# Weights requested in half pieces; ScalarE and VectorE take a tile's round trip in another order

## The reference

```
a   = softmax(q k^T / 8, kept: 4 sink keys and a window of 128) v     # 2 x 8 heads, 768 tokens, head size 64
h   = x @ w_in;  y = (h - tanh(h)) @ w_out                             # 1536 tokens, 512 -> 2048 -> 512
gate: top 2 of 8 experts by x@w_gate + log1p(exp(x@w_noise)) * noise
out[token] += weight * (relu(x @ w1[e]) @ w2[e])                       # per expert 512 -> 1024 -> 512
```

## Time and profile before

| | |
|---|---|
| runs shown | 790.99, 787.76 and 791.50 us; median 790.99 |
| profiled execution, its own time | 789.29 us |
| its span (first to last instruction) | 787.4 us |
| mean granted TensorE clock | 0.977 of 2.4 GHz |
| busy share of the span | PE 95%, POOL 55%, DVE 45%, ACT 29% |
| mean DMA rate | 156 GB/s, 122.48 MB in all |

### The profile page before, as it was taken

How to read it: one execution, slowest core, us unless ns; L and a number is a source line. 1 busy time by engine, 2 the same in 40 slices (tenths; PEclk the granted TensorE clock), 3 DMA queues, 4 the chain that set the end, 5 groups by cost and what they waited for, 6 DMA issues and landing times.

```text
span 787.4 us, 12786 instructions
## 1 busy us (share of the span) xinstructions
PE 746.5 (95%) x3884; PEld 624.8 (79%) x3885; DVE 358.1 (45%) x879; ACT 229.1 (29%) x528; POOL 436.4 (55%) x240
## 2 busy tenths in 40 slices
PE   7999999999999999999987999989998989999884
PEld 6677898898989999998875887868776878888763
DVE  4777533234323523444653444444453535444425
ACT  5999522223223223322311211112111111211100
POOL 6888995000200300069699679297937887803662
PEclk9999999999999999999998999999999999999996
DMA  8542492000200100053636476757657575636748
GB/s 296 221 136 90 141 358 97 1 1 0 81 1 0 71 9 0 0 188 119 260 105 237 149 252 212 263 190 240 213 173 281 182 271 197 216 130 194 218 144 286
DMA packets 59837, 122.48 MB, mean 156 GB/s; under 512 B 6689, under 2 KB 21665, under 8 KB 59809
## 3 DMA queue, kind: packets, MB, share of 16 engines
q1 hardware_dynamic: 28128, 63.92, 22.8%
q10 hardware_dynamic: 27840, 45.62, 17.5%
q0 software_dynamic: 3840, 12.59, 4.7%
HBM read 82.26 MB, written 39.85 MB: 155 GB/s over the span
## 4 chain that ended last, share of the span: by engine, by line
PE 80%; DMA 11%; DVE 3%; issue 2%; ACT 2%; POOL 1%; ACTq 0%; DVEq 0%; POOLq 0%
PE bank L1449 17%; PE bank L1399 17%; PE bank L1542 17%; PE bank L1571 16%; DMA hid_by_lane<-hid 8%; PE bank L1352 4%; PE bank L1343 3%; DMA hid_lanes<-hid_by_lane 3%; PE bank L1325 2%; PE bank L1465 1%; DVE bank L1153 1%; DVE hid L1161 1%; PE bank L1524 1%; PE bank L1459 1%; ACT arena L739 1%
## 5 line engine op out<-in xcount | busy, mean ns | idle before, releaser
L1571 PE MATMUL bank<-ring,hidT_hi 128*128 (+1 forms) x496 | 165.1, 415 | 17.9 <-DVE hidT_lo L1174 13.7
L634 POOL TENSOR_TENSOR ring<-ring_raw,ones 128x2048 fp32r<-128x2048 f32 x32 | 116.0, 3624 | 61.9 <-DMA ring_raw<-in_moe_w 61.8
L636 POOL TENSOR_TENSOR ring<-ring_raw,ring 128x2048 fp32r<-128x2048 f32 x32 | 148.0, 4624 | 2.5
L1542 PE MATMUL bank<-ring,xsT_hi 128*128 (+1 forms) x496 | 135.6, 396 | 7.7 <-DVE hid L1161 6.7
L682 POOL DMA_INDIRECT sorted_x<-y_rows,arena x24 | 25.3, 1053 | 204.6 <-DVEq L1097 198.5
L1571 PEld LDWEIGHTS bank<-ring,hidT_hi 128*128 128x128 f32 x496 | 95.3, 197 | 41.4 <-issue 20.0
L1449 PE MATMUL bank<-w_out_sb,gated_hi 128*128 128x512 f32 x384 | 121.1, 397 | 0.0
L1542 PEld LDWEIGHTS bank<-ring,xsT_hi 128*128 128x128 f32 x496 | 94.0, 191 | 29.2 <-issue 9.5
L1571 PE MATMUL bank<-ring,hidT_lo 128*128 (+1 forms) x248 | 101.2, 408 | 0.0
L1018 DVE TENSOR_TENSOR arena<-bank,arena 128x384 f32<-128x384 f32 x64 | 35.6, 557 | 115.8 <-ACT arena L794 114.8
L1399 PE MATMUL bank<-xT_hi,w_in_hi 128*128 (+1 forms) x256 | 86.7, 339 | 0.0
(11 more groups left out here) (185 smaller groups left out, 993.4 us busy)
## 6 DMA issues: line engine op xcount, KB each, us to landing
ring_raw<-in_moe_w SPq DMA_DIRECT2D x32, 1024.0 KB, 8.4
hid_by_lane<-hid ACTq DMA_DIRECT2D x29, 512.0 KB, 3.1
hid_lanes<-hid_by_lane ACTq DMA_DIRECT2D x29, 512.0 KB, 3.4
sorted_y<-ys ACTq DMA_DIRECT2D x31, 256.0 KB, 3.8
xs<-sorted_x ACTq DMA_DIRECT2D x27, 256.0 KB, 2.8
sorted_y<-zeros SPq DMA_DIRECT2D x1, 4864.0 KB, 25.4
arena<-in_k SPq DMA_DIRECT2D x8, 520.0 KB, 4.1
w_in_raw<-in_moe_w_in SPq DMA_DIRECT2D x2, 2048.0 KB, 9.5
```

Source lines behind the costliest of these rows:

```text
L634: pool.tensor_tensor(hi, raw, one_like(raw), ALU.mult).then_inc(rounded, 1)
L636: ins = pool.tensor_tensor(lo, raw, hi.bitcast(F32), ALU.subtract)
L1542: last = pe.matmul(bank[1 + half][:, :], x[:, c * P:(c + 1) * P], ring[:, bass.ds(at * 2 * WE + (w + c * FE + half * BANK), BANK)], start= ...
L1571: last = pe.matmul(bank[5][:, :], x[:, c * P:(c + 1) * P], ring[:, bass.ds(at * 2 * WE + (w + CH * FE + c * DM), DM)], start=c == 0 and n ...
```

## The change

Four edits. (1) SP requests the first half of a piece, waits until it has landed, requests the second half and waits again; one half piece (512 KB) is under way at a time. The semaphores of the pieces count 32 instead of 16, and POOL waits for both halves. (2) ACT issues `hid_in(t)` as the last thing in `tile(t)`, behind `hid_turned_out(t - 1)` and `store_rows(t - 2)`. (3) DVE turns tile t - 1 inside `tile(t)`, behind `rows_turned_out(t + 1)`, where it had turned tile t at the end of `tile(t)`. (4) The first tiles are written out accordingly: ACT issues `hid_in(2)` behind the input work of tile 4, and DVE turns tile 2 behind the relu of tile 3. What is computed stays the same, and so do the bytes.

```diff
@@ SyncE, for experts 2 to 7
                     sp.wait_ge(used_up, n)
                     dst, src = raw_piece(e, expert, j)
-                    sp.dma_start(dst, src).then_inc(piece_loaded[e % RING][j], 16)
+                    before = 32 * (e // RING - 1)
+                    mid = dst.shape[1] // 2
+                    sp.dma_start(dst[:, 0:mid, :], src[:, 0:mid, :]).then_inc(piece_loaded[e % RING][j], 16)
+                    sp.wait_ge(piece_loaded[e % RING][j], before + 16)
+                    sp.dma_start(dst[:, mid:, :], src[:, mid:, :]).then_inc(piece_loaded[e % RING][j], 16)
+                    sp.wait_ge(piece_loaded[e % RING][j], before + 32)
@@ GpSimd
-                        pool.wait_ge(piece_loaded[e % RING][j], 16 * (e // RING))
+                        pool.wait_ge(piece_loaded[e % RING][j], 32 * (e // RING))
@@ ScalarE, first tiles
             hid_out(2, first=True)
-            hid_in(2, first=True)
             rows_turned_out(4)
             load_rows(5)
+            hid_in(2, first=True)
             relu_out(3)
@@ ScalarE, tile(t)
                     load_rows(t + 2)
-                hid_in(t)
                 hid_turned_out(t - 1, used=t)
                 store_rows(t - 2)
+                hid_in(t)
@@ VectorE, first tiles
             relu_out(2)
-            turn_hidden(2)
...
             relu_out(3, written=True)
+            turn_hidden(2)
             hid_turned_out(2)
-            turn_hidden(3)
@@ VectorE, tile(t), and the end
                 rows_turned_out(t + 1)
+                turn_hidden(t - 1)
                 result_out(t - 2)
                 hid_turned_out(t - 1)
-                turn_hidden(t)
...
+            turn_hidden(TILES - 2)
             result_out(TILES - 3)
```

## The result

The changed kernel takes 764.34 us (median of 4 runs, 762.46 to 765.27), the kernel before 790.43 in the same comparison; the ratio is 0.967, with a 95% interval of 0.964 to 0.970. The forecast was 764.5. On the chips of the later comparisons the kernel before had medians of 787.0 (beside e1 to e4), 788.0 (e5 to e8) and 786.2 us (e9 to e12): the gain was 26.1 us here and 22.4 in e11, the changed kernel once more. Lines of code are 5 higher now: L878 is ACT's relu (L873 before), L865 the write of the hidden values (L860), L873 the read-back (L868), L886 `hidT_hi` (L881), L1158 the transposes (L1153).

The account below looks back on a forecast made before the run. TensorE was taken as nearly always busy, held up when load bursts made writes late and ACT's order passed that on. Steady 17.5, start 7.0 and end 0.7 make 25.2 us: 764.1, forecast 764.5, range 760 to 776.

Parts of the forecast that it names:

- The sum: Whole kernel: gains of steady part, start and end together 25.2 us, giving 764.1 and a forecast of 764.5 us.
- steady part: Passes of the expert stage from 444.91 to 738.71 us: 18.5 us at stake, 17.5 taken as gained, bounds 0 and 18.5.
- start: Around `up(4)`: relu of tile 3 no longer behind tile 2's transposes, 7.0 us gained, bounds 4 and 7.6.
- end: Last tiles: `down(28)` follows `down(27)` at once, idle 2.35 us becomes 1.6, so 0.7 us gained.
- what the new orders do: ACT and DVE loop: with the read-back moved, a write may take 10 us or more; before, ACT fell behind from 5.
- short writes alone: Writes of `hid` beside half pieces: 4 to 6 us, which even the old order would nearly have hidden.
- the moved read-back: `hid_in(t)` issued about U + 7.5, U being the end of `up(t)`: 3.42 us, more likely 4 to 4.5.
- The loads: SP's half pieces of weights: 4.3 us each against 4.9 us free, so loads keep up and POOL is fed.
- the 12 pieces of the prediction's stretch: From the request at 498.59 to expert 6's first `up` at 637.07: 117.7 us for 24 halves, 4.9 us each.
- signs of being wrong: TensorE waiting for POOL's split, or at `up` for DVE's relu or input, or POOL waiting long for `ring_raw`.
- starve POOL: Rival, same stretch: a half takes 5.5 us, 24 take 132, 14.3 more than there is: 779 us; chance 0.08.
- make the loads the bound: Rival, first `up` of expert 6: at 6.5 us a half the loads give 803 us, slower than before; chance 0.04.

Follow-up runs that it names:

- e1: The changed kernel with whole 1 MB pieces requested as before, keeping the new ScalarE and VectorE orders: 780.5 us, ratio 0.993 to the kernel before.
- e4: The kernel before with only ScalarE's loop changed, the read-back issued behind the roundings and the store: 796.9 us, ratio 1.015 to the kernel before.
- e5: The kernel before with only VectorE's new order, in loop and first tiles; whole pieces, old ScalarE order: 778.9 us, ratio 0.986.
- e8: The changed kernel with TensorE itself turning the last tile's hidden values, without their write and read-back: 760.97 us, ratio 0.966 to the kernel before.
- e9: The changed kernel without ScalarE's part: half pieces and VectorE's new order, ScalarE's old order: 764.5 us, ratio 0.972 to the kernel before.
- e12: The changed kernel with TensorE turning the last tile's hidden values, measured again beside the changed kernel: 762.66 us, ratio 0.969 to the kernel before.
- e11: The changed kernel once more, unedited, on the chip of the last comparisons: 763.84 us, ratio 0.970 to the kernel before.
- e2: The kernel before with only half pieces requested one at a time, old ScalarE and VectorE orders: 782.0 us, ratio 0.994 to the kernel before.
- e3: The kernel before with only VectorE's first tiles edited, tile 2 turned behind the relu of tile 3: 787.45 us, ratio 1.002 to the kernel before.
- e7: The changed kernel with quarter pieces of 256 KB, one at a time: 820.29 us, ratio 1.043 to the kernel before.
- e6: The changed kernel with whole 1 MB pieces, one at a time: 768.85 us, ratio 0.975 to the kernel before.

## Why the prediction was right, and where it was not

**The sum.** The change gained 27.1 us of span. By its terms, forecast and measured: steady part 17.5 and 17.2 (18.36 less 1.14); start 7.0 and 7.35 (14.07 less 6.72); end 0.7, and 2.25 from tick 29 to tick 30 (21.22 to 18.97). The rest, 0.3, lies before the tick of tile 2 and after the last tick. Of the end, 0.7 is the shorter pause (2.35 to 1.63) as worked out; the other 1.5 us is the clock, which I had left out. After 1.63 us of pause the stretch has a granted clock of 1.00, where it had been 0.77 (747.1 to 754.4 us in the kernel before):

```profile
721.30:728.00 6.70, 6.70 (x29) 5.47 (x30) 3.32 (x4) 0.00 (x0) 6.70 (x8) 1.00 0.37 120
```

In e11 the pause is 1.94 us, the clock 0.77 in the same stretch, and the pass 1.9 us longer (20.85): this term comes and goes. That forecast and median lie 0.2 us apart is luck: the gain in span was 27.1 us against 25.2 forecast, and by medians 26.1 here and 22.4 in e11.

**The step that failed: what the new orders do.** The prediction said that ACT's order is what makes a late write TensorE's matter, that with the read-back moved a write may take 10 us or more, and that short writes alone would nearly have been hidden in the old order. The first is right and not the whole: e5 shows that wait, ahead of `down`, behind writes of 8.5 and 10.0 us. The other two are wrong. e1 has the new orders and late writes and loses 12.9 us. The prediction had taken 3.4 to 4.5 us for the moved read-back; issued into a burst it took 7.6, ACT stood for it, and the load of the input tile behind it, which the prediction does not mention, landed late for TensorE. e2 has short writes and the old orders and loses 13.7 us, in a circle that the prediction did not count: there is one `hid`, one `hid_by_lane` and one `hid_lanes`, so write, read-back, and in the old order also transposes and relu, follow one another before the next write can go out. e9 shows that ACT's move is worth nothing that could be measured beside the other two.

What the runs show in its place: VectorE's order takes the transposes and the relu, 2.9 us, out of the circle, and halves hold a write to 5.5 and a read-back to 6.2 us. With halves and the old order the circle was 13.29 us against a pass of 11.48 (e2); in the kernel before it sets the time once, from the write at 556.32 (8.54 us, read-back 3.85) to the next at 571.98. With whole pieces and the transposes out of the circle, single transfers of 7.6 to 10 us reach TensorE by whatever stands behind them in ACT's order, the rounding (e5) or the input tile (e1). The single gains in the steady part are 4.7 (e2) and 5.5 (e1), together 10.2; both at once gain 17.2. The medians say the same: 5.0 (e2) and 6.5 us (e1) against 22.4 (e11). I got the sum right because I credited the pair with everything; my reasons would have credited either alone with nearly as much.

**The start** was worked out for tile 4 alone. `up(4)` begins 1 us after `up(3)`, as forecast, in e3 too; that it stays won is the work of the halves, which the prediction did not say. With whole pieces the chain runs through the circle here: in e5 the write of 421.93 takes 8.73 and the read-back 3.27 us, and TensorE waits 2.4 us one tile later.

**The loads.** Forecast were 4.3 us a half against 4.9 free, and no wait. A half landed after 4.4 us (median), and TensorE waited all the same, 0.89 us at 616.09. The chain of the changed kernel ahead of it (start us, us, what):

```profile
563.70 5.61 PE bank L1576 x24
...
569.48 4.11 DMA ring_raw<-in_moe_w
...
582.30 5.56 DMA ring_raw<-in_moe_w
...
588.42 0.88 SPq L571
...
589.76 4.07 DMA ring_raw<-in_moe_w
...
603.10 4.26 DMA ring_raw<-in_moe_w
```

Two things that the prediction did not count stand in it. SP reads its table only behind the last wait of an expert, which takes 1.9 us from 587.86 to 589.76. And the 12 pieces of the prediction's stretch are not one stretch: from 480 to 620 us SP also waited for TensorE (total us, times, longest us):

```profile
SPq L579 <- PE bank L1576: 12.6, 2, 9.2
```

The shorter of the two, 3.4 us, ends at 569.31: pieces 2 and 3 of expert 5 can't be requested before the last `down` of expert 3 is over. What binds is therefore the four passes from there to the first `up` of expert 6, with 8 halves, the table and the last split. From the request at 569.48 to the last landing at 607.36 it is 37.9 us, and 37.0 were free; less 1.9 for the table that is 4.4 us a half, not 4.9. The halves took 4.5 each, request to request, one of them 5.6. A wait for a split ahead of an expert's first `up` is one of the signs of being wrong that the prediction listed; it cost 1.1 us. The rivals that starve POOL or make the loads the bound were given 0.08 and 0.04; their place was right, their threshold too generous, and the kernel sits on the true one: TensorE waited 0.9 and 1.0 us there in two executions (after, e9) and not in e11, and with quarters 55 us are lost in the steady part. The fit that the prediction quotes from the Trainium skill, "DMA: Bandwidth & Descriptors", section "Anatomy of one DMA", is stated there for DMAs that GpSimd issues; SP's halves took 4.4 us where the estimate from it was 3.2.

## What to carry to other kernels

When a loop passes its data through single buffers, count the circle of waits as a whole, and compare it with the pass. When an instruction is moved away from a late transfer, price what then stands behind it, every transfer in the queue included: a wait that one edit removes comes back under another name as long as the late transfer is there. Splitting a large transfer bounds what a small one beside it can wait, and spreads the load over more passes; that pays only where the small one's usual, slightly longer time still fits. Of three edits made together one was worth nothing here, and only leaving out each in turn, with and without the others, showed which.

## What the runs showed of the hardware

A transfer of 512 KB from HBM to SBUF by SP landed after 4.4 us in the median of the changed kernel (3.2 to 5.8), one of 256 KB after 2.9 (e7) and one of 1 MB, alone under way on SP's side, after 6.2 (e6). A 512 KB write issued by ACT, another engine, could take the longer the larger these loads were. The longest write took 11.2 us with whole pieces requested two at a time (before), 7.2 with whole pieces one at a time (e6), 5.5 with halves (after) and 4.5 with quarters (e7); the median moved only from 3.1 to 3.6. A read-back of the same size took 7.6 us behind two whole pieces (e1).

After a pause of 1.63 us TensorE kept its full granted clock (after), and after 1.89 and 1.94 us it ran at 0.77 in the mean of the next 7.5 and 7.3 us (e9, e11). The length of the last pause alone does not decide it: in e5 the clock was 1.00 after a pause of 1.82 us at 515.58 and 0.74 after one of 1.81 at 637.65; in e1 it was 0.79 after two pauses of 1.11 and 1.29 us with the transposes between them, and 1.00 after two of 1.25 and 1.29 at 640.08.
